# Three buffers for the stacked q and k operands, and the output's halves added on GpSimd

## The chip, the core and the metric

The kernel runs on one core of a Trainium2 chip. Its engines are TensorE (PE in the rows), VectorE (DVE), ScalarE (ACT), GpSimd (POOL) and SyncE (SP), which issues most DMAs; each works through its own list of instructions in order, and semaphores tie the lists together. The metric is the device time of one execution in microseconds (us), lower is better.

## The reference, cut to what matters

The whole computation is an attention with bucket masks, then a Fourier-mixing block with an MLP, then a second mixing block. The change touches the attention alone:

```python
B, H, S, D = q.shape                       # 2, 8, 768, 64
scale = 1.0 / np.sqrt(D)
q_bits = (np.einsum('bhsd,dk->bhsk', q, proj) > 0)   # 6 bits a row
k_bits = (np.einsum('bhsd,dk->bhsk', k, proj) > 0)
...
mask = q_bucket[:, :, :, None] == k_bucket[:, :, None, :]
scores = scale * np.matmul(q, k.transpose(0, 1, 3, 2))
scores = np.where(mask, scores, -1000000000.0)
attn = np.exp(scores - np.max(scores, axis=-1, keepdims=True))
attn = attn / (np.sum(attn, axis=-1, keepdims=True) + 1e-09)
return np.matmul(attn, v).astype(np.float32)
```

There are 16 heads (2 x 8) of 768 rows. Its output, laid out as 1,536 rows of 512, is the input X of the rest.

## The kernel before, in words

**Precision.** TensorE works in fp32r; for accuracy each operand is split into a high part (a rounded copy) and a low part (the rest), and products are made of them. For a head, QK holds q transposed in its upper 64 partitions and k transposed in its lower 64. `scale_q` (L492) multiplies the q half by 1/8 on GpSimd. `split_top` makes the stacked operands from it, also on GpSimd: TOPH, the high part (a cast, L500), and TOPL, the low part (a subtraction, L502). SyncE then moves pieces of them (`move_away`, L410 and L411; `move_in`, L417 and L418) so that TOPL, TOPH, QM and KM hold what the score products need.

**Bits and masks.** Six random projections give the bucket bits: unit "bits" of a head (L723 to L725, three matmuls for each half of 384 columns) needs TOPH and TOPL. ScalarE copies the signs out (MB, L642), GpSimd turns them into mask rows (MR, L507), and SyncE sends them into rows 64 to 75 of QM and KM (L426, L427), where the score product takes them as further terms.

**Slots.** The attention runs in slots, one for each of the 96 query tiles of 128 rows, 6 to a head. `schedule` writes the list, and every engine's program walks it. In slot n TensorE does, in this order: the scores of tile n (L770, L771); the transposes of the exponentials of tile n-2 (units eta and etb, L745, three transposes each); two of the six steps of the value product of the head before (L785, L786), whose third part ends a group of three tiles; and then the units of the slot. Those are: in slots 0 and 1 of head h the two "bits" units of head h+1, and in slots 3 and 5 the two "back" units of head h-1, which transpose its output (OS) back into rows (L756). VectorE takes the row maxima (L992) and the exponent's scale and bias (L995) and the low parts of the transposed exponentials (ETL, L1002); ScalarE takes the exponentials (E, L625), the high parts (ETH, L618) and the copies of the value product (OS, L634).

**Output.** A value product carries the high and the low part of v side by side, so that a "back" unit leaves 3 blocks of 128 columns whose two halves of 64 have to be added. ScalarE copies the second halves into OL2 (L647); VectorE adds a constant to the sums (L1022), takes the reciprocals (L1024), and adds the first halves from the bank to OL2 (L1028), all of this for each of the two units of a head. GpSimd's `finish` multiplies by the reciprocals into X (L515). A bank of the ring of three is free when the addition has run.

**GpSimd's order** is what the change moves. In the slots of head h its list holds: slot 0 `finish(h-2, 1)`; slot 1 `mask_rows(h+1)`; slot 2 `split_v(h+1)` (L531, L533), which waits until the value product of head h-1 has ended, then `scale_q(h+2)`; slot 3 `finish(h-1, 0)`; slot 5 `split_top(h+2)`. The "bits" of head h+2 come up on TensorE at the end of slot 0 of head h+1. In the first eight heads GpSimd also issues 16 DMAs for tables and weights, one in slot 2 and one in slot 4 (L560).

Of the kernel before, what the change touches and what calls it, by code (L numbers as in the profile page):

```python
# [5 lines left out]
F32 = mybir.dt.float32  # L6
# [5 lines left out]
P = 128  # L12
# [55 lines left out]
def program(nc, qk, v, projb, w1, w2, wth, wtr, wti, wch, ident_in, gamma_in, sign_in, cs_in, ss_in, alt_in, cd_in, sd_in, out):  # L68
# [35 lines left out]
    OL2 = put("OL2", [P, 2, HALF, D], F32, tail - 4 * 2 * DM)  # L104
    OS2 = put("OS2", [P, 2, HALF, D])
# [21 lines left out]
    XL = put("XL", [1, LC], F32R)  # L127
    used[0] = dft_at + 4 * 4 * QT * KC
# [6 lines left out]
    TOPH = put("TOPH", [P, 2, S], F32R)  # L135
    TOPL = put("TOPL", [P, 2, S], F32R)
# [58 lines left out]
    with ctx:  # L195
# [30 lines left out]
        for u in units:  # L226
# [22 lines left out]
                   "back": sem("s_sum")}  # L249
        s_ol = sem("s_ol")  # L250
# [137 lines left out]
        def _(sp):  # L388
# [16 lines left out]
            def move_away(h):  # L405
                b = h % 2
                sp.wait_ge(s_top, 2 * (h + 1))
                if h >= 2:
                    sp.wait_ge(s_s, QT * (h - 1))
                sp.dma_start(QM[0:D, b].bitcast(F32), TOPH[0:D, b].bitcast(F32)).then_inc(s_away, 16)  # L410
                sp.dma_start(KM[0:D, b].bitcast(F32), TOPL[D:P, b].bitcast(F32)).then_inc(s_away, 16)  # L411

            def move_in(h):
                b = h % 2
                sp.wait_ge(s_ring, done["bits", h, 1])
                sp.wait_ge(s_away, 32 * (h + 1))
                sp.dma_start(TOPL[D:P, b].bitcast(F32), QM[0:D, b].bitcast(F32)).then_inc(s_in, 16)  # L417
                sp.dma_start(TOPH[0:D, b].bitcast(F32), TOPH[D:P, b].bitcast(F32)).then_inc(s_in, 16)  # L418

# [55 lines left out]
        def _(pool):  # L475
# [18 lines left out]
            def split_top(h):  # L494
                b = h % 2
                pool.wait_ge(s_sq, h)
                pool.wait_ge(s_top, 2 * h)
                if h >= 2:
                    pool.wait_ge(s_s, QT * (h - 1))
                nc.gpsimd.tensor_copy(TOPH[:, b], QK[:, b]).then_inc(s_top, 1)  # L500
                pool.wait_ge(s_top, 2 * h + 1)
                nc.gpsimd.tensor_tensor(TOPL[:, b], QK[:, b], TOPH[:, b].bitcast(F32), ALU.subtract).then_inc(s_top, 1)  # L502
# [6 lines left out]
            def finish(h, i):  # L509
                first, half = h * QT + i * HALF, 2 * h + i  # L510
                st = slice(first % NSTAT, first % NSTAT + HALF)
                row = (h // H) * QT + i * HALF
                pool.wait_ge(s_inv, 2 * half + 2)
                pool.wait_ge(emptied["back"], half + 1)
                nc.gpsimd.tensor_tensor(X[:, row:row + HALF, (h % H) * D:(h % H + 1) * D], OS2[:, i],  # L515
# [22 lines left out]
            for slot, (tile, et, pv, us) in enumerate(slots):  # L538
# [15 lines left out]
                if slot and t == 3 and h:  # L554
                    finish(h - 1, 0)
                if slot and t == 5 and h + 2 < NH:
                    split_top(h + 2)
                if slot and t in (2, 4) and early:
# [33 lines left out]
        def _(act):  # L592
# [16 lines left out]
            for slot, (tile, et, pv, us) in enumerate(slots):  # L609
# [25 lines left out]
                for u in us:  # L635
# [7 lines left out]
                    elif kind == "back":  # L643
                        act.wait_ge(s_ring, done[u])
                        if h:
                            act.wait_ge(emptied["back"], nth[u] - 2)
                        nc.scalar.activation(OL2[:, i], blocks(ring(unit_no[u])[:, 0:HC])[:, :, D:P], ACT.Copy).then_inc(s_ol, 1)  # L647

# [71 lines left out]
        def _(pe):  # L720
# [12 lines left out]
            def unit(name):  # L733
# [12 lines left out]
                elif kind == "bits":  # L746
# [5 lines left out]
                    last = product(bank[0:2 * NM, 0:HC], projH[:], TOPH[:, h % 2, c], projL[:], TOPL[:, h % 2, c], True, True)  # L752
# [6 lines left out]
            for tile, et, pv, us in slots:  # L759
                if tile is not None:  # L760
# [7 lines left out]
                    for lo, hi in ((0, 512), (512, S)):  # L768
                        dst = s_bank(tile)[:, lo:hi]
                        nc.tensor.matmul(dst, TOPL[:, h % 2, c], TOPH[:, h % 2, lo:hi], start=True, stop=False)  # L770
# [170 lines left out]
        def _(dve):  # L941
# [44 lines left out]
            for slot, (tile, et, pv, us) in enumerate(slots):  # L986
# [23 lines left out]
                for u in us:  # L1010
# [234 lines left out]
```

## Time and profile before

| what | value |
|---|---|
| median of 3 runs | 849.54 us (846.16 to 853.26) |
| profiled execution | 848.04 us |
| its span | 845.3 us |
| mean granted TensorE clock | 0.96 |
| TensorE busy | 752.8 us (89%) |
| VectorE busy | 455.6 us (54%) |
| ScalarE busy | 318.4 us (38%) |
| GpSimd busy | 268.0 us (32%) |

The attention ends at about 315 us of the span. The page's line of slices (40 equal slices of 21 us) shows TensorE at 7 to 8 tenths there and at 9 after it, with a granted clock of 0.8 to 0.9 of full speed in most slices up to the eighth, and full speed from then to the end of the attention:

```profile
PE   3788888888888876979999999999997899999998
DVE  2667677778899987863221212121115656765433
POOL 2655555565656306734500000020001122321200
PEclk9889899999999997789999999999998999999999
```

The chain that ended last gives TensorE 75% of the span and GpSimd 12%; GpSimd's largest lines in it are L492 (4%) and L502 (3%).

### The profile page before, as it was taken

The numbers are of one execution on the slowest core, as the hardware profiler recorded it, in microseconds if no ns is written. First come the engines' busy times: TensorE is split into PE (matmuls) and PEld (weight loads), VectorE is DVE, ScalarE is ACT, GpSimd is POOL, SyncE is SP. The second block draws the span as 40 slices with busy tenths as digits, with TensorE's granted clock in tenths as the row PEclk, the third lists the DMA queues.
The fourth block names the chain that finished last, engine by engine and source line by source line (L and its number), as shares of the span: only waits on it lengthen the run. The fifth ranks groups of instructions, "written<-read, shape, count | busy, mean of one in ns | idle before, by whom it ended". The sixth has DMA issues, their size and how long they took to land.

```text
span 845.3 us, 11003 instructions
## 1 busy us (share of the span) xinstructions
PE 752.8 (89%) x3826; PEld 629.7 (74%) x3826; DVE 455.6 (54%) x834; ACT 318.4 (38%) x659; POOL 268.0 (32%) x243
## 2 busy tenths in 40 slices
PE   3788888888888876979999999999997899999998
PEld 2677777777877865768888888888885687888876
DVE  2667677778899987863221212121115656765433
ACT  2667667777877851111111111101113343231301
POOL 2655555565656306734500000020001122321200
PEclk9889899999999997789999999999998999999999
DMA  5343443553332103372200000220002222000001
GB/s 144 82 124 90 104 111 94 169 169 93 103 83 70 42 1 112 113 224 75 74 1 1 1 0 1 63 76 0 1 1 70 69 61 88 0 13 13 26 26 74
DMA packets 44680, 56.26 MB, mean 67 GB/s; under 512 B 15956, under 2 KB 27860, under 8 KB 44116
## 3 DMA queue, kind: packets, MB, share of 16 engines
q1 hardware_dynamic: 38100, 41.65, 17.8%
q0 software_dynamic: 6528, 13.92, 5.7%
q8 instruction: 32, 0.52, 0.3%
q14 instruction: 20, 0.16, 0.1%
HBM read 38.65 MB, written 3.15 MB: 49 GB/s over the span
## 4 chain that ended last, share of the span: by engine, by line
PE 75%; POOL 12%; DVE 5%; issue 3%; ACT 2%; DMA 1%; SPq 1%; POOLq 0%; ACTq 0%
PE PS L723 19%; PE PS L725 18%; PE PS L724 18%; PE PS L745 5%; POOL QK L492 4%; POOL TOPL L502 3%; PE PS L770 3%; PE PS L785 3%; PE PS L771 3%; PE PS L786 3%; POOL TOPH L500 1%; PE PS L906 1%; POOL VHL L531 1%; PE PS L913 1%; POOL VHL L533 1%
## 5 line engine op out<-in xcount | busy, mean ns | idle before, releaser
L1117 DVE SCALAR_TENSOR_TENSOR HL<-PS,HH 128x512 fp32r<-128x512 f32 x48 | 33.2, 692 | 186.6 <-ACT HH L686 186.6
L992 DVE TENSOR_REDUCE negmax<-PS 128x1 f32<-128x768 f32 x96 | 91.3, 951 | 59.9 <-PE PS L771 59.9
L625 ACT ACTIVATE E<-PS,affine 128x768 f32<-128x768 f32 x96 | 95.4, 994 | 39.7 <-DVE affine L995 38.2
L686 ACT ACTIVATE HH<-PS 128x512 fp32r<-128x512 f32 x48 | 28.7, 598 | 208.9 <-PE PS L725 208.9
L1002 DVE TENSOR_TENSOR ETL<-PS,ETH 128x384 fp32r<-128x384 f32 x192 | 97.9, 548 | 0.9 <-ACT ETH L618 0.5
L618 ACT ACTIVATE ETH<-PS 128x384 fp32r<-128x384 f32 x192 | 84.3, 489 | 24.5 <-PE PS L745 22.8
L745 PE MATMUL PS<-ident,E 128*128 128x128 f32 x576 | 84.5, 282 | 1.2
L785 PE MATMUL PS<-ETH,VHL 128*128 128x384 f32 x192 | 75.1, 391 | 8.9 <-ACT OS L634 6.3
L723 PE MATMUL PS<-UTH,W1H 128*128 128x512 f32 x192 | 76.2, 397 | 1.7 <-DVE UTL L1100 1.7
L770 PE MATMUL PS<-TOPH,TOPL 128*128 128x512 f32 x192 | 70.3, 366 | 6.7 <-DMA KM<-MR 6.0
L725 PE MATMUL PS<-UTH,W1L 128*128 128x512 f32 x192 | 75.3, 392 | 0.0
L724 PE MATMUL PS<-UTL,W1H 128*128 128x512 f32 x192 | 75.2, 392 | 0.0
L725 PE MATMUL PS<-W2H,HL 128*128 128x512 f32 x192 | 74.7, 389 | 0.0
L723 PE MATMUL PS<-W2H,HH 128*128 128x512 f32 x192 | 74.7, 389 | 0.0
L724 PE MATMUL PS<-W2L,HH 128*128 128x512 f32 x192 | 74.7, 389 | 0.0
L745 PEld LDWEIGHTS PS<-ident,E 128*128 128x128 f32 x576 | 68.2, 145 | 3.8 <-DVE ETL L1002 3.5
L507 POOL TENSOR_SCALAR MR<-MB,gamma 24x768 fp32r<-24x768 f32 x15 | 43.9, 2930 | 77.8 <-ACT MB L642 77.8
L786 PE MATMUL PS<-ETL,VHL 128*128 128x384 f32 x192 | 66.9, 348 | 0.0
L586 POOL TENSOR_TENSOR ZF<-X,SC 128x512 f32<-128x512 f32 x24 | 30.5, 1290 | 106.0 <-ACT SC L707 106.0
L771 PE MATMUL PS<-KM,QM 76*128 76x512 f32 x192 | 63.5, 351 | 0.0
L723 PE MATMUL PS<-ZH,WTH 128*128 128x512 f32 x144 | 59.2, 411 | 0.0
L725 PE MATMUL PS<-ZH,WTL 128*128 128x512 f32 x144 | 56.5, 392 | 0.0
(167 smaller groups left out, 1525.6 us busy)
## 6 DMA issues: line engine op xcount, KB each, us to landing
stage<-in_moe_w_ch_dram SPq DMA_DIRECT2D x36, 256.0 KB, 2.6
QK<-in_qk_dram SPq DMA_DIRECT2D x16, 384.0 KB, 3.9
W1H<-in_moe_w_ch_dram POOLq DMA_DIRECT2D x4, 1024.0 KB, 8.2
W2H<-in_moe_w_ch_dram POOLq DMA_DIRECT2D x4, 1024.0 KB, 8.9
QM<-TOPH SPq DMA_DIRECT2D x16, 192.0 KB, 2.8
KM<-TOPL SPq DMA_DIRECT2D x16, 192.0 KB, 3.1
TOPL<-QM SPq DMA_DIRECT2D x16, 192.0 KB, 2.7
TOPH<-TOPH SPq DMA_DIRECT2D x16, 192.0 KB, 3.0
```

The lines of the kernel that those rows point to most:

```text
L618: nc.scalar.activation(ETH[:, t // HALF, k * HALF:(k + 1) * HALF, (t % HALF) * P:(t % HALF + 1) * P], bank, ACT.Copy).then_inc(s_eth, 1)
L625: nc.scalar.activation(E[:, tile % NE, :], s_bank(tile)[:, 0:S], ACT.Exp, bias=affine[:, t, 1:2], scale=affine[:, t, 0:1], accum_out=esum[ ...
L723: nc.tensor.matmul(dst, hl, hr, start=start, stop=False)
L724: nc.tensor.matmul(dst, hl, lr, start=False, stop=False)
L725: return nc.tensor.matmul(dst, ll, hr, start=False, stop=stop)
L745: last = nc.tensor.transpose(bank[:, j * P:(j + 1) * P], E[:, tile % NE, (first + j) * P:(first + j + 1) * P], ident[:])
L770: nc.tensor.matmul(dst, TOPL[:, h % 2, c], TOPH[:, h % 2, lo:hi], start=True, stop=False)
L771: last = nc.tensor.matmul(dst, QM[:, h % 2, c], KM[:, h % 2, lo:hi], start=False, stop=True)
L785: nc.tensor.matmul(OT, VHL[:, h % 2, j, :], ETH[:, c, j, :], start=(j == 0), stop=False)
L786: last = nc.tensor.matmul(OT, VHL[:, h % 2, j, :], ETL[:, c, j, :], start=False, stop=(j == QT - 1))
L992: nc.vector.tensor_reduce(negmax[:, t, 1:2], s_bank(tile)[:, 0:S], AX_X, ALU.max, negate=True).then_inc(s_max, 1)
L1002: nc.vector.tensor_tensor(ETL[where], blocks(ring(unit_no[kind, h, t])[:, 0:HC]), ETH[where].bitcast(F32), ALU.subtract).then_inc(emptied[ ...
```

## The change

- TOPH and TOPL get a third buffer, and a head's parts are in buffer h % 3. `split_top(h)` on GpSimd then waits for the scores of head h-3 where it waited for those of head h-2. QK, QM and KM keep two.
- `split_top(h+2)` stands in slot 3 of head h where it stood in slot 5, and the second DMA of GpSimd in slot 5 where it stood in slot 4.
- ScalarE copies both halves of a "back" unit (128 x 384) into OL2, which sets the bank free.
- GpSimd adds the halves in `finish`, ahead of the multiplication, and waits for its own addition between them. VectorE's addition is gone.
- VectorE takes the reciprocals of a head's six columns at once, with the first "back" unit.

```diff
-    OL2 = put("OL2", [P, 2, HALF, D], F32, tail - 4 * 2 * DM)
-    OS2 = put("OS2", [P, 2, HALF, D])
+    OL2 = put("OL2", [P, 2, HALF, P], F32, tail - 4 * 2 * DM)
+    OS2 = put("OS2", [P, HALF, D])
...
             def move_away(h):
-                b = h % 2
+                b, r = h % 2, h % 3
                 sp.wait_ge(s_top, 2 * (h + 1))
                 if h >= 2:
                     sp.wait_ge(s_s, QT * (h - 1))
-                sp.dma_start(QM[0:D, b].bitcast(F32), TOPH[0:D, b].bitcast(F32)).then_inc(s_away, 16)
-                sp.dma_start(KM[0:D, b].bitcast(F32), TOPL[D:P, b].bitcast(F32)).then_inc(s_away, 16)
+                sp.dma_start(QM[0:D, b].bitcast(F32), TOPH[0:D, r].bitcast(F32)).then_inc(s_away, 16)
+                sp.dma_start(KM[0:D, b].bitcast(F32), TOPL[D:P, r].bitcast(F32)).then_inc(s_away, 16)
...
             def split_top(h):
-                b = h % 2
+                b, r = h % 2, h % 3
                 pool.wait_ge(s_sq, h)
                 pool.wait_ge(s_top, 2 * h)
-                if h >= 2:
-                    pool.wait_ge(s_s, QT * (h - 1))
-                nc.gpsimd.tensor_copy(TOPH[:, b], QK[:, b]).then_inc(s_top, 1)
+                if h >= 3:
+                    pool.wait_ge(s_s, QT * (h - 2))
+                nc.gpsimd.tensor_copy(TOPH[:, r], QK[:, b]).then_inc(s_top, 1)
                 pool.wait_ge(s_top, 2 * h + 1)
-                nc.gpsimd.tensor_tensor(TOPL[:, b], QK[:, b], TOPH[:, b].bitcast(F32), ALU.subtract).then_inc(s_top, 1)
+                nc.gpsimd.tensor_tensor(TOPL[:, r], QK[:, b], TOPH[:, r].bitcast(F32), ALU.subtract).then_inc(s_top, 1)
...
             def finish(h, i):
-                first, half = h * QT + i * HALF, 2 * h + i
-                st = slice(first % NSTAT, first % NSTAT + HALF)
+                half = 2 * h + i
+                st = slice((half * HALF) % NSTAT, (half * HALF) % NSTAT + HALF)
                 row = (h // H) * QT + i * HALF
-                pool.wait_ge(s_inv, 2 * half + 2)
                 pool.wait_ge(emptied["back"], half + 1)
-                nc.gpsimd.tensor_tensor(X[:, row:row + HALF, (h % H) * D:(h % H + 1) * D], OS2[:, i],
+                if half:
+                    pool.wait_ge(s_x, half)
+                nc.gpsimd.tensor_tensor(OS2[:], OL2[:, i, :, 0:D], OL2[:, i, :, D:P], ALU.add).then_inc(s_sum, 1)
+                pool.wait_ge(s_sum, half + 1)
+                pool.wait_ge(s_inv, 2 * (h + 1))
+                nc.gpsimd.tensor_tensor(X[:, row:row + HALF, (h % H) * D:(h % H + 1) * D], OS2[:],
                                         einv[:, st].unsqueeze(2).to_broadcast([P, HALF, D]), ALU.mult).then_inc(s_x, 1)
...
-                if slot and t == 3 and h:
-                    finish(h - 1, 0)
-                if slot and t == 5 and h + 2 < NH:
-                    split_top(h + 2)
-                if slot and t in (2, 4) and early:
+                if slot and t == 3:
+                    if h:
+                        finish(h - 1, 0)
+                    if h + 2 < NH:
+                        split_top(h + 2)
+                if slot and t in (2, 5) and early:
...
                         if h:
-                            act.wait_ge(emptied["back"], nth[u] - 2)
-                        nc.scalar.activation(OL2[:, i], blocks(ring(unit_no[u])[:, 0:HC])[:, :, D:P], ACT.Copy).then_inc(s_ol, 1)
+                            act.wait_ge(s_sum, nth[u] - 2)
+                        nc.scalar.activation(OL2[:, i], blocks(ring(unit_no[u])[:, 0:HC]), ACT.Copy).then_inc(emptied["back"], 1)
...
-                    elif kind == "back":
-                        first, half = h * QT + i * HALF, 2 * h + i
-                        st = slice(first % NSTAT, first % NSTAT + HALF)
-                        dve.wait_ge(s_exp, first + HALF)
+                    elif kind == "back" and i == 0:
+                        st = slice(h * QT % NSTAT, h * QT % NSTAT + QT)
+                        dve.wait_ge(s_exp, (h + 1) * QT)
                         nc.vector.tensor_scalar(einv[:, st], esum[:, st], 1e-9, None, ALU.add).then_inc(s_inv, 1)
-                        dve.wait_ge(s_inv, 2 * half + 1)
+                        dve.wait_ge(s_inv, 2 * h + 1)
                         nc.vector.reciprocal(einv[:, st], einv[:, st]).then_inc(s_inv, 1)
-                        dve.wait_ge(s_ol, nth[u])
-                        if h:
-                            dve.wait_ge(s_x, nth[u] - 2)
-                        nc.vector.tensor_tensor(OS2[:, i], blocks(bank[:, 0:HC])[:, :, 0:D], OL2[:, i], ALU.add).then_inc(emptied["back"], 1)
```

**GpSimd's list, one head.** From the split of v for head 2 to the first mask row after it, in head 1 of the attention. Before:

```order
L531 CAST VHL<-VR 128x6x64 [waits s_pv,s_v0]
L533 TENSOR_TENSOR VHL<-VR,VHL 128x6x64 [waits s_vs]
L492 TENSOR_SCALAR QK<-QK 64x768 [waits s_qk1]
L560 DMA CSH<-in_cs_dram 128x3x386
L515 TENSOR_TENSOR X<-OS_68,einv 128x3x64 [waits s_sum,s_inv]
L560 DMA SSH<-in_ss_dram 128x3x386
L500 CAST TOPH<-QK 128x768 [waits s_s,s_top,s_sq]
L502 TENSOR_TENSOR TOPL<-QK,TOPH 128x768 [waits s_top]
L515 TENSOR_TENSOR X<-OS_68,einv 128x3x64 [waits s_sum,s_inv]
L507 TENSOR_SCALAR MR<-MB,gamma 24x768 [waits s_mask,s_bits]
```

The same piece of the changed kernel (its lines are four or five further down):

```order
L535 CAST VHL<-VR 128x6x64 [waits s_pv,s_v0]
L537 TENSOR_TENSOR VHL<-VR,VHL 128x6x64 [waits s_vs]
L492 TENSOR_SCALAR QK<-QK 64x768 [waits s_qk1]
L565 DMA CSH<-in_cs_dram 128x3x386
L516 TENSOR_TENSOR OS_68<-OL_67 128x192 [waits s_ol]
L519 TENSOR_TENSOR X<-OS_68,einv 128x3x64 [waits s_inv,s_sum]
L500 CAST TOPH<-QK 128x768 [waits s_s,s_top,s_sq]
L502 TENSOR_TENSOR TOPL<-QK,TOPH 128x768 [waits s_top]
L565 DMA SSH<-in_ss_dram 128x3x386
L516 TENSOR_TENSOR OS_68<-OL_67 128x192 [waits s_x,s_ol]
```

The two instructions of `split_top` have the same neighbours as before but for two: the second DMA is behind them, and an addition (OS_68<-OL_67) stands ahead of them. In heads without DMAs the addition is the only difference.

**VectorE's list around the two "back" units of a head.** Before:

```order
L1002 TENSOR_TENSOR ETL<-PS,ETH 128x3x128 [waits s_eth] x2
L1022 TENSOR_SCALAR einv<-esum 128x3 [waits s_exp]
L1024 RECIPROCAL einv<-einv 128x3 [waits s_inv]
L1028 TENSOR_TENSOR OS_68<-PS,OL_67 128x192 [waits s_x,s_ol]
L992 TENSOR_REDUCE negmax<-PS 128x1 [waits s_s]
```

The changed kernel, at the first unit of a head:

```order
L1007 TENSOR_TENSOR ETL<-PS,ETH 128x3x128 [waits s_eth] x2
L1026 TENSOR_SCALAR einv<-esum 128x6 [waits s_exp]
L1028 RECIPROCAL einv<-einv 128x6 [waits s_inv]
L997 TENSOR_REDUCE negmax<-PS 128x1 [waits s_s]
L1000 SCALAR_TENSOR_TENSOR affine<-negmax 128x2 [waits s_max]
```

The addition and its wait for ScalarE are gone from in front of the row maximum; at the second unit nothing is left but the pair of ETL and the maximum.

## Rows read from the trace of the kernel before

**Rows 1.** Stretches from a head's bits to its v split: us, busy by engine, clock, DMA.

```profile
core 0: us, PE busy (x) PEld busy (x) DVE busy (x) ACT busy (x) POOL busy (x), PEclk, DMA share, GB/s
33.60:46.35 12.75, 12.75 (x67) 11.37 (x68) 7.87 (x17) 8.27 (x18) 2.93 (x1) 0.76 0.41 106
75.78:87.30 11.52, 11.52 (x67) 10.40 (x68) 7.73 (x17) 8.27 (x18) 3.25 (x2) 0.85 0.46 116
95.77:108.19 12.42, 12.42 (x67) 11.08 (x68) 7.87 (x17) 8.27 (x18) 3.25 (x3) 0.78 0.41 108
154.73:166.26 11.53, 11.53 (x67) 10.49 (x68) 7.86 (x17) 8.27 (x18) 3.25 (x2) 0.85 0.71 200
174.47:184.42 9.95, 9.95 (x67) 9.14 (x68) 7.71 (x16) 7.93 (x18) 3.25 (x2) 1.00 0.75 212
191.40:201.35 9.95, 9.95 (x67) 9.16 (x68) 8.53 (x18) 8.80 (x20) 3.25 (x2) 1.00 0.51 127
```

**Rows 2.** The same view, stretches from a v split to the next bits.

```profile
46.35:55.05 8.70, 4.58 (x32) 3.90 (x31) 6.07 (x14) 5.48 (x12) 8.50 (x9) 0.90 0.49 120
166.26:174.47 8.21, 4.57 (x32) 3.90 (x30) 6.09 (x14) 5.48 (x12) 8.01 (x9) 1.00 0.51 157
218.28:225.26 6.98, 4.79 (x31) 3.88 (x30) 6.78 (x14) 4.38 (x11) 6.81 (x7) 1.00 0.13 30
```

**Rows 3.** Timeline of GpSimd, a late head: start us, us, what [idle before <-releaser].

```profile
218.28 0.50 POOL L531 CAST VHL<-VR 128x384 fp32r<-128x384 f32 x1 [2.49 <-PE PS L786]
218.87 1.01 POOL L533 TENSOR_TENSOR VHL<-VR,VHL 128x384 fp32r<-128x384 f32 x1
219.85 2.13 POOL L492 TENSOR_SCALAR QK<-QK 64x768 f32<-64x768 f32 x1
221.96 0.50 POOL L515 TENSOR_TENSOR X<-OS,einv 128x192 f32<-128x192 f32 x1
222.42 0.81 POOL L500 CAST TOPH<-QK 128x768 fp32r<-128x768 f32 x1
223.31 1.80 POOL L502 TENSOR_TENSOR TOPL<-QK,TOPH 128x768 fp32r<-128x768 f32 x1
```

**Rows 4.** Timeline of GpSimd, a head with DMA issues.

```profile
170.56 0.52 POOL L515 TENSOR_TENSOR X<-OS,einv 128x192 f32<-128x192 f32 x1
171.01 0.59 POOL L560 DMA_DIRECT2D W1H<-in_moe_w_ch_dram  x1
171.60 0.84 POOL L500 CAST TOPH<-QK 128x768 fp32r<-128x768 f32 x1
```

**Rows 5.** Timeline of TensorE, instructions that end an idle time.

```profile
136.56 0.34 PE L723 MATMUL PS<-TOPH,projH 128*24 128x384 f32 x1 [3.17 <-POOL TOPL L502]
154.73 0.34 PE L723 MATMUL PS<-TOPH,projH 128*24 128x384 f32 x1 [2.73 <-POOL TOPL L502]
220.44 0.41 PE L785 MATMUL PS<-ETH,VHL 128*128 128x384 f32 x1 [0.57 <-ACT OS L634]
225.26 0.33 PE L723 MATMUL PS<-TOPH,projH 128*24 128x384 f32 x1 [1.49 <-POOL TOPL L502]
```

**Rows 6.** Timeline of VectorE and ScalarE around a "back" unit.

```profile
298.93 0.32 ACT L647 ACTIVATE OL<-PS 128x192 f32<-128x192 f32 x1
299.28 0.36 DVE L1028 TENSOR_TENSOR OS<-PS,OL 128x192 f32<-128x192 f32 x1 [0.15 <-ACT OL L647]
299.48 0.87 ACT L618 ACTIVATE ETH<-PS 128x384 fp32r<-128x384 f32 x2 [0.24 <-PE PS L745]
300.73 0.99 ACT L625 ACTIVATE E<-PS,affine 128x768 f32<-128x768 f32 x1 [0.37 <-DVE affine L995]
```

**Rows 7.** Timeline of VectorE beside the TOPL of Rows 3.

```profile
223.54 1.60 DVE L995 SCALAR_TENSOR_TENSOR affine<-negmax 128x2 f32<-128x2 f32 x1
```

**Rows 8.** Timeline of SyncE and TensorE: the mask rows of a head, and its first scores.

```profile
164.09 0.77 SPq L427 DMA_DIRECT2D KM<-MR  x1
...
169.02 0.48 PE L770 MATMUL PS<-TOPH,TOPL 128*128 128x512 f32 x1
```

**Rows 9.** The page's DMA issues: KB of each, median us to landing.

```profile
KM<-TOPL SPq DMA_DIRECT2D x16, 192.0 KB, 3.1
```

More of the change, by code:

```diff
@@ L127, in program @@
     XL = put("XL", [1, LC], F32R)
+    TOPL = put("TOPL", [P, 3, S], F32R)
     used[0] = dft_at + 4 * 4 * QT * KC
@@ L134, in program @@
     work_at = used[0]
-    TOPH = put("TOPH", [P, 2, S], F32R)
-    TOPL = put("TOPL", [P, 2, S], F32R)
+    TOPH = put("TOPH", [P, 3, S], F32R)
     QM = put("QM", [D + NM, 2, S], F32R)
@@ L248, in program @@
                    "pv": sem("s_os"),
-                   "back": sem("s_sum")}
-        s_ol = sem("s_ol")
+                   "back": sem("s_ol")}
+        s_sum = sem("s_sum")
         s_x = sem("s_x")
@@ L409, in move_away @@
                     sp.wait_ge(s_s, QT * (h - 1))
-                sp.dma_start(QM[0:D, b].bitcast(F32), TOPH[0:D, b].bitcast(F32)).then_inc(s_away, 16)
-                sp.dma_start(KM[0:D, b].bitcast(F32), TOPL[D:P, b].bitcast(F32)).then_inc(s_away, 16)
+                sp.dma_start(QM[0:D, b].bitcast(F32), TOPH[0:D, r].bitcast(F32)).then_inc(s_away, 16)
+                sp.dma_start(KM[0:D, b].bitcast(F32), TOPL[D:P, r].bitcast(F32)).then_inc(s_away, 16)
             def move_in(h):
-                b = h % 2
+                b, r = h % 2, h % 3
                 sp.wait_ge(s_ring, done["bits", h, 1])
                 sp.wait_ge(s_away, 32 * (h + 1))
-                sp.dma_start(TOPL[D:P, b].bitcast(F32), QM[0:D, b].bitcast(F32)).then_inc(s_in, 16)
-                sp.dma_start(TOPH[0:D, b].bitcast(F32), TOPH[D:P, b].bitcast(F32)).then_inc(s_in, 16)
+                sp.dma_start(TOPL[D:P, r].bitcast(F32), QM[0:D, b].bitcast(F32)).then_inc(s_in, 16)
+                sp.dma_start(TOPH[0:D, r].bitcast(F32), TOPH[D:P, r].bitcast(F32)).then_inc(s_in, 16)
             def move_mask(h):
@@ L494, in split_top @@
             def split_top(h):
-                b = h % 2
+                b, r = h % 2, h % 3
                 pool.wait_ge(s_sq, h)
                 pool.wait_ge(s_top, 2 * h)
-                if h >= 2:
-                    pool.wait_ge(s_s, QT * (h - 1))
-                nc.gpsimd.tensor_copy(TOPH[:, b], QK[:, b]).then_inc(s_top, 1)
+                if h >= 3:
+                    pool.wait_ge(s_s, QT * (h - 2))
+                nc.gpsimd.tensor_copy(TOPH[:, r], QK[:, b]).then_inc(s_top, 1)
                 pool.wait_ge(s_top, 2 * h + 1)
-                nc.gpsimd.tensor_tensor(TOPL[:, b], QK[:, b], TOPH[:, b].bitcast(F32), ALU.subtract).then_inc(s_top, 1)
+                nc.gpsimd.tensor_tensor(TOPL[:, r], QK[:, b], TOPH[:, r].bitcast(F32), ALU.subtract).then_inc(s_top, 1)
             def mask_rows(h):
@@ L751, in unit @@
                         pe.wait_ge(s_proj, 3)
-                    last = product(bank[0:2 * NM, 0:HC], projH[:], TOPH[:, h % 2, c], projL[:], TOPL[:, h % 2, c], True, True)
+                    last = product(bank[0:2 * NM, 0:HC], projH[:], TOPH[:, h % 3, c], projL[:], TOPL[:, h % 3, c], True, True)
                 elif kind == "back":
@@ L769, in _ @@
                         dst = s_bank(tile)[:, lo:hi]
-                        nc.tensor.matmul(dst, TOPL[:, h % 2, c], TOPH[:, h % 2, lo:hi], start=True, stop=False)
+                        nc.tensor.matmul(dst, TOPL[:, h % 3, c], TOPH[:, h % 3, lo:hi], start=True, stop=False)
                         last = nc.tensor.matmul(dst, QM[:, h % 2, c], KM[:, h % 2, lo:hi], start=False, stop=True)
```

## The prediction, as made before the changed kernel ran

> **What bounds the kernel now.** I read the page first, for the chain that ended last: outside the attention it is TensorE almost alone, and the change leaves that part as it is. Inside the attention GpSimd's L492 and L502 stand in it, so there TensorE waits for a slower partner. The timeline of GpSimd in a late head shows how. Its v split starts when TensorE's last value product of the head before has ended, after 2.49 us of waiting for it; then the split, the scaling (2.13), the multiplication into X (0.50), the cast to TOPH (0.81) and the subtraction to TOPL (1.80) follow without a break [rows 3]. TensorE's bits of the next head wait for TOPL: 1.49 us idle at 225.26 [rows 5]. So a head is a closed loop of two stretches, and I cut the trace at these two points with the view of busy time by stretch. From the bits to the v split TensorE is busy all the time, 9.95 us at a clock of 1.00 [rows 1]. From the v split to the bits GpSimd is busy for 6.81 of 6.98 us, and TensorE for 4.79 [rows 2]. The sum is 16.93 us, a late head's period. The reader is to see that only two things change a period: what GpSimd does in the second stretch, and TensorE's clock in the first.
>
> Both differ in the first eight heads. The second stretch takes 8.70 us in the first that has all its parts and 8.21 in the last; seven such stretches take 8.41 on average, since two DMA issues stand in them [rows 2, 4]. And the first stretch takes 9.95 us in two of these eight heads, 11.52 or 11.53 in three, and 12.3 to 12.8 in three, at mean clocks of 0.85 and 0.76 to 0.79 [rows 1]: the granted clock fell to the lower of its two levels, 1.2 GHz, after TensorE had stood idle. Above 9.95 the eight add up to 12.4 us. An idle time of 2.73 us was followed by a fall (the stretch from 154.73, clock 0.85), one of 3.17 was not, and one of 1.49 was not [rows 1, 5].
>
> **The third buffer and the earlier slot.** They remove a wait of `split_top` for scores of the head before the last. That wait is not what holds it: the cast starts the moment the multiplication ahead of it has ended, with no idle time on GpSimd [rows 3]. In GpSimd's list `split_top` keeps its place behind the v split and the scaling, so "two heads ahead" is what it was before. It still cannot start before the last value product of the head before. Worth nothing by itself; what hides it is the list's order. SyncE's moves wait for TOPL and for QM and KM, which keep two buffers, and so stay where TOPL puts them.
>
> **The second DMA behind TOPL.** This one is off the loop now. The two issues cost 8.41 - 6.98 = 1.43 us, one half 0.71 (the issue itself shows 0.59 [rows 4]). Seven heads give 5.0 us, and the first head another 0.5: **-5.5 us**. Behind TOPL it fills time in which GpSimd waits for its mask rows anyway.
>
> **The addition on GpSimd.** The first `finish` of a head stands in the second stretch, ahead of TOPH and TOPL. The nearest rows for its addition (two inputs in SBUF, 128 x 192) are the multiplication of the same size, 0.50, and half of the 128 x 384 subtraction, 0.50 [rows 3]. The multiplication now waits for it, and where one GpSimd instruction waits for another's result the rows show 0.08 us between them (218.78 to 218.87, 223.23 to 223.31). So 0.58 us; the bounds are 0.36, VectorE's time for the same addition [rows 6], and 1.01, should it cost what twice the size does. Thirteen stretches have it (seven with DMAs, six without): 13 x 0.58 = **+7.5 us**, with bounds of 4.7 and 13. The second `finish` runs behind TOPL, in idle time, and costs nothing. The Trainium skill, "GPSIMD Engine Reference", section "Engine selection", speaks against the move: it wants elementwise work with two inputs on VectorE and calls GpSimd about twice as slow. By that factor on VectorE's 0.36 the addition would take 0.72 and the sum would be 2 us higher; here the same-sized row of 0.50 decides.
>
> **VectorE's relief.** In slots 3 and 5 the row maximum no longer stands behind the addition, which ended at 299.64 and held the maximum up. The exponential after it then goes when ScalarE is free, at the end of ETH (299.48 + 0.87 = 300.35) where it went at 300.73: 0.38 us earlier [rows 6]. ScalarE's longer copy (about 0.48 for 128 x 384, where it was 0.32) still ends before that ETH starts. The copy OS and the value product behind it come 0.38 earlier, so that TensorE's idle of 0.57 [rows 5] shrinks to some 0.2. But inside the loop this shortens nothing: TensorE merely reaches the wait for TOPL sooner. Only the last two heads, which have no split left to wait for, gain it: 2 x 0.38, less 0.15 for the longer copy at the end: **-0.6 us**. The reciprocals once a head are in the same place, off the path.
>
> **The clock.** The wait for TOPL grows. In the six late heads it was 1.49; it becomes 1.49 + 0.58 + 0.38 = 2.45 us. No row shows such a length. Of the neighbours, 1.49 never cost the clock, 2.73 did once, 3.17 did not once. So bound it by no fall and six falls, and take three, because 2.45 is nearer to 2.73 and even longer gaps were let off. A fall costs 11.53 - 9.95 = 1.58 us [rows 1]: **+4.7 us**, with bounds of 0 and 9.5. In the early heads the gap is 0.13 shorter by GpSimd and 0.38 longer by VectorE's relief; I take half a fall more than now, **+0.8**. The Trainium skill, "TensorE: Matmul & The Clock Gate", section "Why this matters for your kernels", has a rule of thumb by which idle gaps of 2.45 us would be harmless; by it the two clock terms would be nothing. The trace's fall after 2.73 us is against it, and that is the first rival.
>
> **A port.** VectorE's small L995 took 1.60 us beside GpSimd's TOPL, and ended with it [rows 7], where it takes 0.16 alone. The Trainium skill, "SBUF — State Buffer", section "Who interferes with whom", calls that an exclusive lock of the two engines. The addition brings more of it, but it falls into the stretch where TensorE waits for TOPL in any case, so I cost it at nothing.
>
> **The sum** is made against the profiled execution, 848.04 us, which is 1.5 below the median: 848.0 - 5.5 + 7.5 - 0.6 = 849.4 without the clock, and + 4.7 + 0.8 = **855 us**. About 1% (8.5 us) is what a measurement of this kernel can tell from no change: up to 858.0 and down to 841.0.
>
> **The rivals.**
> - *The clock stays up* in the late heads, or falls once: 849.4 to 851, no change. For it: 3.17 us was let off. Against it: 2.73 was not. Chance 0.25.
> - *The clock falls in five or six late heads, and in all early ones*: 849.4 + 9.5 + 2 x 1.6 to 2 x 2.5, or 862 to 864; with an addition of nearly 1.01 us, 868. For it: six of eight early gaps were followed by a fall. Chance 0.18.
> - *The other side: the early heads keep their clock.* The issue that leaves the loop is worth up to 0.8 us in the heads with the large tables, and if the addition took only 0.36, the early gaps would shrink by 0.3 to 0.4. Should that let all six early falls go, while 2.3 us in the late heads is harmless, the time would be 849.4 - 2.8 - 12.4 = 834; with four of the six gone 838. It decides from early gaps of under 2.7 us, and these stand at 2.73 to 3.65. Chance 0.06.
> - *A late DMA.* The second weight transfer (1 MB) goes out behind TOPL, together with SyncE's moves. The mask rows of a head were issued until 164.86 and the scores that need them started at 169.02 [rows 8], 4.2 us for a transfer of some 3.1 us [rows 9]. If the moves come 3 us later in two or three heads, TensorE waits some 2 us in each and the clock may fall as well: 859 to 861. Chance 0.04.
> - The forecast, two to four falls in the late heads, 852 to 858: chance 0.47.
>
> **How the numbers follow.** The likeliest is 855. The range runs from 848, which takes in the case of no fall with a cheaper addition, to 864, which takes in most of the case of all falls. Slower by over 1%: 0.18 + 0.04 and a fifth of the forecast's own 0.47 at its upper end, 0.31. Faster by over 1%: 0.06 and 0.01 for what is not thought of: 0.07. The rest, 0.62, is within 1%.
>
> **What would show it.** In the profile after: the stretch from the v split to the bits at 7.56 us in late heads and about 8.3 in early ones; L516 at 0.50 ahead of each TOPH; TensorE's wait for TOPL near 2.4 us; the value product of slot 5 waiting 0.2 instead of 0.57; first stretches of 11.5 us among the late heads, where there were none. The prediction is wrong if GpSimd idles ahead of TOPH in the trace of before after all (it does not in these rows), if the late period falls below 16.9 us, or if the time after the attention differs.

## The result: 2.7% slower

The changed kernel took 870.58 us (median of 4 runs, 868.66 to 876.39) against 847.85 us of the kernel before on the same chip (4 runs, 844.84 to 853.26): a ratio of 1.0272, with an interval of [1.0196, 1.0348]. The forecast was 855 us with a range up to 864. The profiled execution took 868.66 us, its span 866.6 us, its mean granted clock 0.933 where it had been 0.96.

The stretches of the changed kernel, cut as in [rows 1]: from a head's bits to the next v split. The first four are early heads, the others late ones.

```profile
core 0: us, PE busy (x) PEld busy (x) DVE busy (x) ACT busy (x) POOL busy (x), PEclk, DMA share, GB/s
32.42:44.97 12.55, 12.55 (x67) 11.20 (x68) 8.00 (x17) 8.71 (x19) 3.29 (x3) 0.77 0.41 105
74.30:85.84 11.54, 11.54 (x67) 10.47 (x68) 7.92 (x17) 8.70 (x19) 4.46 (x4) 0.85 0.51 127
135.63:147.12 11.49, 11.49 (x67) 10.38 (x68) 7.84 (x17) 8.70 (x19) 4.45 (x5) 0.85 0.54 128
176.22:188.60 12.38, 12.38 (x67) 11.06 (x68) 8.02 (x17) 8.69 (x19) 4.43 (x4) 0.79 0.74 185
...
196.29:206.23 9.94, 9.94 (x67) 9.14 (x68) 7.85 (x17) 8.13 (x19) 3.84 (x4) 1.00 0.52 127
...
231.45:243.00 11.55, 11.55 (x67) 10.47 (x68) 8.02 (x17) 8.70 (x19) 3.84 (x4) 0.85 0.45 114
...
250.67:263.33 12.66, 12.66 (x67) 11.31 (x68) 8.01 (x17) 8.70 (x19) 3.84 (x3) 0.77 0.40 105
...
291.36:304.15 12.79, 12.79 (x67) 11.38 (x68) 8.01 (x17) 8.69 (x19) 3.84 (x3) 0.76 0.28 67
```

No early stretch is at 9.95 us any more: two of the eight read 11.5 us and six read 12.2 to 12.6 (all eight add up to 97.5 us, where it was 92.0). Of the six late ones, which all read 9.95 before, one reads 11.55 and three 12.66 to 12.79. The number of instructions (x67 on TensorE) is the same; only the clock (0.76 to 0.85) differs.

The stretches from a v split to the next bits, which answer to [rows 2]:

```profile
core 0: us, PE busy (x) PEld busy (x) DVE busy (x) ACT busy (x) POOL busy (x), PEclk, DMA share, GB/s
44.97:53.52 8.55, 4.58 (x31) 3.90 (x30) 5.36 (x10) 5.15 (x12) 8.28 (x9) 0.90 0.34 89
167.93:176.22 8.29, 4.58 (x32) 3.90 (x30) 5.78 (x10) 5.27 (x12) 8.02 (x9) 0.91 0.45 145
206.23:213.88 7.65, 4.57 (x32) 3.90 (x31) 5.56 (x10) 5.45 (x12) 7.41 (x8) 1.00 0.12 29
263.33:270.98 7.65, 4.59 (x32) 3.91 (x31) 5.70 (x10) 5.26 (x12) 7.40 (x8) 0.95 0.08 19
```

In early heads GpSimd's stretch is what it was (8.39 on average, where it was 8.41), in late ones it is 7.65 where it was 6.98. In the last row the clock is already down inside the gap (0.95 on average; in steps of 1 us it reads 1.00 up to 270 us and 0.64 from 270 to 271, the last step before the bits). GpSimd's timeline of a late head, against [rows 3]:

```profile
206.23 0.50 POOL L535 CAST VHL<-VR 128x384 fp32r<-128x384 f32 x1 [2.47 <-PE PS L791]
206.81 1.00 POOL L537 TENSOR_TENSOR VHL<-VR,VHL 128x384 fp32r<-128x384 f32 x1
207.79 2.14 POOL L492 TENSOR_SCALAR QK<-QK 64x768 f32<-64x768 f32 x1
209.91 0.59 POOL L516 TENSOR_TENSOR OS<-OL 128x192 f32<-128x192 f32 x1
210.58 0.51 POOL L519 TENSOR_TENSOR X<-OS,einv 128x192 f32<-128x192 f32 x1
211.03 0.82 POOL L500 CAST TOPH<-QK 128x768 fp32r<-128x768 f32 x1
211.93 1.80 POOL L502 TENSOR_TENSOR TOPL<-QK,TOPH 128x768 fp32r<-128x768 f32 x1
```

The chain is the old one with L516 in it, 0.67 us from its start to the multiplication's. On TensorE, against [rows 5], the value product of slot 5 hardly waits, and the wait for TOPL has nearly doubled:

```profile
207.71 0.41 PE L790 MATMUL PS<-ETH,VHL 128*128 128x384 f32 x1 [0.24 <-ACT OS L639]
213.88 0.33 PE L728 MATMUL PS<-TOPH,projH 128*24 128x384 f32 x1 [2.83 <-POOL TOPL L502]
250.67 0.49 PE L728 MATMUL PS<-TOPH,projH 128*24 128x384 f32 x1 [3.00 <-POOL TOPL L502]
```

The spans differ by 21.3 us (866.6 and 845.3). Summed over the stretches of the two profiles:

| part | difference, us | forecast |
|---|---|---|
| up to the first v split, and the first head's short stretch | -1.2 | -0.5 |
| v split to bits, seven early | -0.2 | -0.9 |
| v split to bits, six late | +4.1 | +3.5 |
| bits to v split, eight early (clock) | +5.5 | +0.8 |
| bits to v split, six late (clock) | +9.9 | +4.7 |
| last value products of the attention | -0.9 | -0.6 |
| behind the attention | +4.1 | 0 |

The last row is mostly the clock as well. I read the granted clock behind the last value product in steps of 2 us: the time at the lower level adds up to 37.5 us in the kernel before and to 44.4 in the changed one. By TensorE's busy time in those steps that is some 3.7 of the 4.1 us, an estimate.

### The profile page after: what moved, and what is told of

It is laid out like the page before. It is cut to its first block, busy times and chain, and to the rows that moved or that the text cites. A ratio compares the mean times of both kernels' runs of the same rounds, so it can differ in the third digit from the quotient of the medians.

```text
span 866.6 us, 10972 instructions
## 1 busy us (share of the span) xinstructions
PE 769.5 (89%) x3826; PEld 644.4 (74%) x3826; DVE 440.3 (51%) x770; ACT 325.2 (38%) x659; POOL 287.5 (33%) x275
## 4 chain that ended last, share of the span: by engine, by line
PE 77%; POOL 12%; DVE 4%; issue 3%; DMA 1%; ACT 1%; SPq 1%; POOLq 0%; ACTq 0%
PE PS L728 19%; PE PS L729 18%; PE PS L730 18%; PE PS L750 6%; POOL QK L492 3%; PE PS L775 3%; PE PS L790 3%; PE PS L776 3%; PE PS L791 3%; POOL TOPL L502 3%; POOL TOPH L500 1%; PE PS L911 1%; POOL OS L516 1%; POOL VHL L535 1%; PE PS L918 1%
## 5 line engine op out<-in xcount | busy, mean ns | idle before, releaser
L750 PE MATMUL PS<-ident,E 128*128 128x128 f32 x576 | 86.9, 290 | 0.1
L790 PE MATMUL PS<-ETH,VHL 128*128 128x384 f32 x192 | 77.6, 404 | 2.6 <-ACT OS L639 1.2
L775 PE MATMUL PS<-TOPH,TOPL 128*128 128x512 f32 x192 | 72.9, 380 | 7.0 <-DMA KM<-MR 6.0
L750 PEld LDWEIGHTS PS<-ident,E 128*128 128x128 f32 x576 | 71.6, 149 | 1.1 <-DVE ETL L1007 0.8
L791 PE MATMUL PS<-ETL,VHL 128*128 128x384 f32 x192 | 69.1, 360 | 0.0
L776 PE MATMUL PS<-KM,QM 76*128 76x512 f32 x192 | 65.9, 362 | 0.0
L728 PE MATMUL PS<-TOPH,projH 128*24 128x384 f32 x32 | 14.8, 462 | 52.6 <-POOL TOPL L502 46.7
```

The costliest lines, as they stand in the source:

```text
L728: nc.tensor.matmul(dst, hl, hr, start=start, stop=False)
L750: last = nc.tensor.transpose(bank[:, j * P:(j + 1) * P], E[:, tile % NE, (first + j) * P:(first + j + 1) * P], ident[:])
L775: nc.tensor.matmul(dst, TOPL[:, h % 3, c], TOPH[:, h % 3, lo:hi], start=True, stop=False)
L776: last = nc.tensor.matmul(dst, QM[:, h % 2, c], KM[:, h % 2, lo:hi], start=False, stop=True)
L790: nc.tensor.matmul(OT, VHL[:, h % 2, j, :], ETH[:, c, j, :], start=(j == 0), stop=False)
L791: last = nc.tensor.matmul(OT, VHL[:, h % 2, j, :], ETL[:, c, j, :], start=False, stop=(j == QT - 1))
```

## The experiments

Each was timed in three rounds (seven to nineteen runs of the kernel before beside it). The theory: GpSimd's list sets the loop, and the idle time it leaves TensorE lowers the granted clock, which is most of the loss. The rival: the work itself, the port or the new buffers cost the time. The kernel before was timed beside each group of experiments, and its median was 847.4 to 850.4 us; so kernels of different groups are better compared by their ratios to it.

**Keep TensorE busy in the gap.** Two kernels, the changed one and the one before (there with `% 2`), with `K` matmuls of no use:

```diff
                 elif kind == "bits":
                     c = slice(i * HC, (i + 1) * HC)
+                    if h >= 2 and i == 0:
+                        for _ in range(K):
+                            nc.tensor.matmul(bank[0:2 * NM, 0:HC], projH[:], TOPH[:, (h - 1) % 3, 0:HC], start=True, stop=True)
                     pe.wait_ge(s_top, 2 * (h + 1))
```

> The changed kernel with matmuls of no use ahead of TensorE's wait for TOPL (16 in the eight heads with DMAs, 12 in the late ones; each 128*24 by 384, written to the bits' bank, which the bits then overwrite). Clock theory: most of the loss is the granted clock. No first stretch (bits to v split) is over 10.1 us, the clock in them 1.00; the second stretches stay at 8.3 to 8.5 and 7.65, since GpSimd sets their length; 15.5 us for the eight early and 9.9 us for the six late stretches come back: about 841 to 846 us, faster than the kernel before. Rival, that the falls are not caused by the idle time, or that the longer GpSimd list is the whole loss: the falls stay or go over to another place, and the time stays at 865 to 870 us.

> The kernel before with the same kind of matmuls (14 in the early heads, 6 in the late ones). Clock theory: the six falls of the early heads (12.4 us over eight stretches) go, nothing else changes: 834 to 838 us. The difference between this kernel and the changed one with its filler is then the change without its clock: the second stretches (+4.1 late, -0.7 early), start and end (-1.5), +1 to +4 us. Rival (the change costs much more than these stretches): a difference of over 8 us stays between the two.

Measured: 840.86 us for the changed kernel (ratio to the kernel before 0.9913 [0.9876, 0.9950]) and 835.90 us for the kernel before (0.9868 [0.9822, 0.9913]). So with 200 matmuls more (16 in each of eight heads, 12 in each of six), the changed kernel is 30 us faster than without them; the kernel before gains 12 with 148 (14 and 6). Here a first stretch begins with the first of these matmuls. An early and a late head of the changed kernel with them:

```profile
core 0: us, PE busy (x) PEld busy (x) DVE busy (x) ACT busy (x) POOL busy (x), PEclk, DMA share, GB/s
156.89:170.38 13.49, 12.91 (x84) 10.70 (x83) 9.03 (x20) 9.25 (x22) 7.92 (x9) 1.00 0.85 229
170.38:175.04 4.66, 4.41 (x31) 3.95 (x30) 4.42 (x8) 4.33 (x10) 4.50 (x5) 1.00 0.41 101
...
227.71:240.60 12.89, 12.22 (x80) 10.28 (x79) 8.98 (x20) 9.26 (x22) 6.79 (x6) 1.00 0.39 98
240.60:245.26 4.66, 4.42 (x31) 3.96 (x30) 4.42 (x8) 4.33 (x10) 4.49 (x5) 1.00 0.19 44
```

The clock is 1.00 in every stretch of the attention, in both kernels. The late head takes 12.89 + 4.66 = 17.55 us, which is what the changed kernel's takes where its clock does not fall (7.65 + 9.94): the matmuls fill the gap and do not shorten GpSimd's list. What is left between the two kernels with the clock out of the way is 840.86 - 835.90 = 5.0 us, a little above the 1 to 4 expected and far from the rival's 8 or more; the late heads' 0.67 us, six times, would be 4.0 of it. The two profiles are 8.5 us apart, of which 3.2 lie ahead of the last v split (275.68 and 272.49) and 5.3 behind it. So of the 23 us of the loss some 18 go with the clock in the attention, counting what it costs either kernel.

**One more addition on GpSimd, VectorE's left in place.** The kernel before, with an addition of 128 x 192 whose result nobody reads:

```diff
                 pool.wait_ge(emptied["back"], half + 1)
+                if i == 0:
+                    if h:
+                        pool.wait_ge(s_dum, h)
+                    nc.gpsimd.tensor_tensor(DUM[:], OS2[:, i], OS2[:, i], ALU.add).then_inc(s_dum, 1)
+                    pool.wait_ge(s_dum, h + 1)
```

> The kernel before with one more addition of 128x192 on GpSimd ahead of each head's first multiplication, with its wait; its result is not used. VectorE's addition stays. Theory: the late second stretch goes from 6.98 to 7.6 us, the late gap to 1.49+0.6 = 2.1 us (the value product keeps its 0.57 of waiting), the early gaps to 3.3 to 4.2. If the length of the gap decides on the clock, the late heads at 2.1 us lose it less often than those of the changed kernel at 2.9 (0 to 3 of 6, one of them 1.6 us), the early ones all: 13*0.6 = 8 us, +3 to 6 us for the early clock, +0 to 5 for the late one: 859 to 867 us. Rival (the addition is the whole loss, and VectorE's relief has no part in it): the late heads fall as often as in the changed kernel, 4 of 6, most of them for 2.4 us or more: 868 us or more.

Measured: 866.56 us (860.21 to 873.52), 1.0204 [1.0130, 1.0277]. The late stretch from v split to bits is 7.56 us, the gaps of the late heads 2.05 to 2.51 us, and two of the six late heads lose the clock, by 1.6 us each, where the changed kernel loses it in four and for longer. This profile is of the fastest of the four runs, so the others may have lost it more often. The early heads lose it in all eight, as expected, but after gaps of 3.2 to 4.2 us they lose only 1.5 to 1.6 each, 12.5 in all, where it was 12.4 before and 3 to 6 more were expected. So the addition in the loop makes a loss of 2% by itself, 19 of 23 us, though this kernel lacks the gain of the second DMA that the changed one has. By the medians it is 4 us better than the changed kernel, but the intervals overlap; that VectorE's relief makes matters worse shows in the gaps (2.1 to 2.5 against 2.8 to 3.0) and is not clear in the time.

**The addition back on VectorE**, all else as changed:

```diff
-                nc.gpsimd.tensor_tensor(OS2[:], OL2[:, i, :, 0:D], OL2[:, i, :, D:P], ALU.add).then_inc(s_sum, 1)
...
+                        nc.vector.tensor_tensor(OS2[:, i], blocks(bank[:, 0:HC])[:, :, 0:D], OL2[:, i], ALU.add).then_inc(emptied["back"], 1)
```

> The changed kernel with the addition back on VectorE and the narrow copy on ScalarE; the third buffer, the second DMA behind TOPL and the reciprocals once a head stay. Theory: the late second stretches are 6.98 again, the early ones 7.7 (8.41 less 0.7), gaps of about 1.5 to 1.7 in the late heads and 2.2 to 3.0 in the early ones, so that the early falls get fewer: 848 - 5.5 - 0 to 9 = 833 to 843 us. Rival (the third buffer or its place in memory costs something by itself): 850 us or more.

Measured: 838.04 us, 0.9883 [0.9833, 0.9933]. The rest of the change is a gain of 1.2%, so the addition's move costs 3.9% (1.0272 against 0.9883).

**The second DMA behind `split_top`, alone**, in the kernel before:

```diff
-                if slot and t in (2, 4) and early:
+                if slot and t in (2, 5) and early:
```

> The kernel before with the second DMA of a head on GpSimd behind split_top, and nothing else. Theory: early second stretches 7.7 in place of 8.4 us, five and a half us in all, early gaps 2.1 to 3.0 us and fewer falls, 0 to 9 us more: 833 to 843 us, about as e4_after_dve_add, so the third buffer adds nothing to it. Rival (this part of the change is worthless because the transfer comes late): 846 us or more.

Measured: 839.29 us, 0.9886 [0.9824, 0.9948]: the same as the one above, whose profiled stretches it repeats to 0.05 us. So the third buffer and the reciprocals once a head add nothing to it.

**The first `finish` of a head behind `split_top`**, the addition staying on GpSimd:

```diff
                 if slot and t == 3:
-                    if h:
-                        finish(h - 1, 0)
                     if h + 2 < NH:
                         split_top(h + 2)
+                    if h:
+                        finish(h - 1, 0)
```

> The changed kernel with the first finish of a head (addition and multiplication) behind split_top. Theory: 1.07 us leave the loop: late second stretch 7.65-1.07 = 6.58 us, early 7.25, gaps of 1.9 us in late and 2.2 to 2.5 us in early heads; no or few falls: 828 to 842 us. Rival (the addition costs by its port or its work, wherever it stands): 860 us or more.

Measured: 841.10 us, 0.9872 [0.9814, 0.9929]. The late second stretch is 6.62 us. The same addition on the same engine, off the loop, leaves the time at what it is with the addition on VectorE (0.9883). The multiplication left the loop with it, so this does not show that the addition alone costs nothing there. Six of the fourteen heads still lost the clock, two of them late heads after gaps of 1.95 and 1.80 us, which was not expected; the other four late heads kept it after 1.82 to 1.96.

**The length of the gap.** The changed kernel with fewer of the matmuls: `K` of 4 and of 8 in each of the fourteen heads.

> The changed kernel with 4 matmuls of no use ahead of TensorE's wait for TOPL in every head: gaps of 2.9-0.7 = 2.2 us in late heads and 2.9 to 3.2 in early ones; GpSimd's list as in the changed kernel. Theory (the length of the gap sets how often and how long the clock falls): the three falls of 2.7 us in late heads turn into shorter or no falls (0 to 5 us in the six in place of 9.9), the early ones shrink from 17.9 to about 12 us as in the kernel before: 853 to 862 us. Rival (filler of any length does it, or the falls have another cause): 841 to 846 as with 12 to 16 matmuls, or 868 and more.

> The same with 8 matmuls: gaps of 1.5 us in late heads, as in the kernel before, and 2.2 to 2.5 us in early ones. Theory: no falls in the late heads, 2 to 5 single ones in the early heads (0 to 8 us): 842 to 851 us. Rival: the late heads keep falls although their gap is that of the kernel before: 853 us or more.

Measured: 850.35 us (ten runs, 1.0032 [0.9998, 1.0066]) and 847.97 us (ten runs, 0.9974 [0.9935, 1.0013]). The first is 3 us better than expected. The six late heads of six profiles, by the idle time of TensorE ahead of the bits:

| gap of the late heads, us | kernel | heads with a fall | us lost in the six |
|---|---|---|---|
| 0.9 to 1.4 | changed, 8 matmuls | 0 | 0 |
| 1.49 | before | 0 | 0 |
| 1.8 to 2.0 | `finish` behind | 2 | 3.2 |
| 2.0 to 2.2 | changed, 4 matmuls | 2 | 3.1 |
| 2.1 to 2.5 | before, one more addition | 2 | 3.2 |
| 2.8 to 3.0 | changed | 4 | 9.9 |

Longer gaps in the late heads go with more falls, but within one profile the length does not decide: with one more addition the two falls stand behind gaps of 2.05 and 2.06 us, and the two gaps of 2.5 were let off. Nor does it set the price of a fall. In the eight early heads, by the same cut:

| gap of the early heads, us | kernel | heads with a fall | us of one fall |
|---|---|---|---|
| 1.2 to 2.4 | changed, 8 matmuls | 5 | 1.5 to 1.6 |
| 1.9 to 3.1 | changed, 4 matmuls | 5 | 1.6 |
| 2.7 to 3.65 | before | 6 | 1.6 in three, 2.4 to 2.8 in three |
| 3.1 to 3.9 | changed | 8 | 1.5 to 1.6 in two, 2.3 to 2.6 in six |
| 3.2 to 4.2 | before, one more addition | 8 | 1.5 to 1.6 |

The early falls with 4 matmuls cost some 8 us together where about 12 were expected, which accounts for the 3 us by which that kernel was faster than forecast. The profile with 8 matmuls is of one of its longer runs (853.66 us).

**The split ahead of the v split.** Here the three buffers are put to use: in the changed kernel, `scale_q` and `split_top` no longer stand behind the wait for the value product.

```diff
-                    if h + 1 < NH:
-                        split_v(h + 1)
                     if h + 2 < NH:
                         scale_q(h + 2)
+                        split_top(h + 2)
+                    if h + 1 < NH:
+                        split_v(h + 1)
                 if slot and t == 3:
                     if h:
                         finish(h - 1, 0)
-                    if h + 2 < NH:
-                        split_top(h + 2)
```

> The changed kernel with scale_q and split_top of head h+2 moved ahead of split_v(h+1) on GpSimd, so that they no longer wait for the value product of the head before; this is where three buffers allow the parts two heads ahead. Theory of the loop: TOPL of the next head is there before TensorE gets to its bits, TensorE has no wait of over 1 us in the heads, the second stretch falls to TensorE's own 4.8 to 5.2 us and the clock is 1.00: per head 9.95+5.0 = 15 us for 14 heads, some 14*1.9 + 9*0.5 (early DMAs) + 12 = 43 us under the kernel before: 800 to 812 us. Rival (a next wait stands right behind: mask rows or the DMAs of the moves): a new idle time of 1 us or more at L770/L775, 815 to 840 us.

Measured: **800.84 us, 0.9410 [0.9365, 0.9455]**, faster than both kernels. GpSimd's timeline of a late head:

```profile
199.18 2.93 POOL L507 TENSOR_SCALAR MR<-MB,gamma 24x768 fp32r<-24x768 f32 x1 [2.70 <-ACT MB L646]
202.09 2.13 POOL L492 TENSOR_SCALAR QK<-QK 64x768 f32<-64x768 f32 x1
204.29 0.82 POOL L500 CAST TOPH<-QK 128x768 fp32r<-128x768 f32 x1
205.20 1.83 POOL L502 TENSOR_TENSOR TOPL<-QK,TOPH 128x768 fp32r<-128x768 f32 x1
206.98 0.50 POOL L535 CAST VHL<-VR 128x384 fp32r<-128x384 f32 x1
```

The scaling and the split to TOPH and TOPL now follow the mask rows in time in which GpSimd used to wait for the value product, and TOPL is done at 207.03, as the v split starts and 2.2 us ahead of the bits at 209.24. One whole head, v split to v split, in this kernel:

```profile
core 0: us, PE busy (x) PEld busy (x) DVE busy (x) ACT busy (x) POOL busy (x), PEclk, DMA share, GB/s
207.00:221.62 14.62, 14.41 (x98) 13.13 (x97) 13.27 (x28) 13.40 (x30) 11.36 (x12) 1.00 0.39 100
```

TensorE is busy for 14.41 of 14.62 us; the period was 16.93 before and 17.6 to 20.4 in the changed kernel. One early head of this profile takes 17.24 us: VectorE's small L999 takes 1.69 us there (from 129.72) and ends with TOPL at 131.4, and TensorE waits 1.35 us for the ETL behind it, against the expectation of no wait over 1 us.

**The same with two buffers** (`h % 2`, and the wait of the kernel before):

> As e5_split_first, but with two buffers for TOPH and TOPL, so that the cast waits for the last scores of the head before. Theory: the scaling is done early, cast and subtraction (2.7 us) start at the end of slot 5's scores and end about 1 us before the bits: nearly the same as e5, 800 to 815 us, so the order and not the third buffer is what matters. Rival: the wait for the scores binds and the gap before the bits stays at 1 us or more, and the v split behind it comes late: 820 us or more.

Measured: 809.06 us, 0.9506 [0.9462, 0.9551]; the third buffer is worth 8 us here. No wait for TOPL is left, as expected. But the cast now waits for the last scores, TOPL falls beside slot 5, and VectorE's small L999 is held until TOPL has ended (215.71), as L995 was in [rows 7], now with TensorE behind it:

```profile
213.90 1.83 DVE L999 SCALAR_TENSOR_TENSOR affine<-negmax 128x2 f32<-128x2 f32 x1
215.66 1.01 DVE L1006 TENSOR_TENSOR ETL<-PS,ETH 128x384 fp32r<-128x384 f32 x2
```

```profile
213.88 1.83 POOL L502 TENSOR_TENSOR TOPL<-QK,TOPH 128x768 fp32r<-128x768 f32 x1
```

```profile
216.25 1.01 PE L749 MATMUL PS<-ident,E 128*128 128x128 f32 x6 [0.57 <-DVE ETL L1006]
```

A head takes 15.52 us, 0.9 more than with three buffers; this wait is 0.57 of it, and the rest was not followed. The order without the third buffer brings 41 us against the kernel before (the GpSimd addition and the DMA's place are in these 41), the third buffer another 8.

The lock between the two engines is what the Trainium skill, "SBUF — State Buffer", section "Who interferes with whom", states as a rule; the trace agrees, with 1.83 us for an instruction on two elements a partition.

**The addition on VectorE once the loop is gone:**

> e5_split_first with the addition back on VectorE (narrow copy on ScalarE, reciprocals once a head). Theory: with the split out of the loop GpSimd has time to spare (11 of 14.6 us) while VectorE has not (it was busy for 13.3 of 14.6 us), so here the addition is better on GpSimd: VectorE's list grows by 2*0.36 us and its waits for ScalarE, and the period by 0 to 0.7 us: 801 to 811 us. Rival (the engine of the addition does not matter): 801 us as e5.

Measured: 805.84 us, 0.9503 [0.9456, 0.9549], 5 us slower by the medians than with the addition on GpSimd, and 8 by the ratios (0.9503 against 0.9410), since the two were timed in different groups. In every head the value product waits 0.57 us for OS again, and a head takes 15.3 us:

```profile
core 0: us, PE busy (x) PEld busy (x) DVE busy (x) ACT busy (x) POOL busy (x), PEclk, DMA share, GB/s
195.99:211.31 15.32, 14.62 (x97) 13.11 (x97) 13.82 (x29) 13.29 (x32) 10.15 (x9) 1.00 0.38 97
```

**The changed kernel once more**, unchanged:

> The changed kernel once more, unchanged, with its own profile. Theory: the second stretches repeat to 0.1 us (8.3 to 8.5 early, 7.65 late); the falls in the late heads come in another pattern, 3 to 6 of them, together 5 to 13 us; the time after the attention is 559 to 566 us, differing from the first profile by the clock alone. Rival (a cause of the change itself behind the attention): again 3 us more than the 559.3 of the kernel before, with the same clock.

Measured: 869.77 us, 1.0243 [1.0186, 1.0301]. The second stretches repeat. Against the expectation the falls repeat too, head by head; what varies is the time behind the attention, 565.8 us from the last v split where it was 562.5 in the first profile of the same kernel and 559.3 in the kernel before. The time at the lower clock behind the last value product adds up to 51.2 us here, where it was 44.4 and 37.5. So differences of 3 us in that part come without any change, by the clock. That the +4.1 of the table has nothing to do with the change is not shown by this: both profiles of the changed kernel lie above the kernel before, as the rival had it, though not at the same clock. In the profiles of the experiments that part took 560.8 us or more wherever GpSimd did the addition, and 559.4 to 559.9 in three of the five where it did not (the other two 562.3 and 563.8). The cause stays open.

## Why the prediction was wrong, by its own steps

- **What bounds the kernel** was right: the loop of two stretches, with GpSimd's list in one and TensorE's clock in the other, is what every experiment moved.
- **The third buffer is worth nothing by itself** was right (the DMA alone does the same as the DMA, the buffer and the reciprocals together), and so was its reason: `split_top` stands behind a v split that waits. Lifted over it, the buffer is worth 8 us.
- **The second DMA** was forecast at -5.5 us. The table has -0.2 for seven early stretches, out of this gain and the additions; moved alone in the kernel before, the DMA took 0.6 to 0.8 us from each, and with three early falls fewer it came to 1.1%.
- **The addition** was forecast at 0.58 us and measured 0.67 (0.59 and the wait): +4.1 us for +3.5 in the late heads. A small miss; its row was another instruction of the same size.
- **VectorE's relief** was forecast at 0.38 us and was about 0.7. I counted the wait for OS, which shrank from 0.57 to 0.24, and missed the transposes of slot 5: the six ahead of that value product take 0.82 us where the same six took 1.18, and TensorE's busy time of the stretch fell from 4.79 to 4.57 with the same work. Before, and in the changed kernel:

```profile
218.69 1.18 PE L745 MATMUL PS<-ident,E 128*128 128x128 f32 x6
206.65 0.82 PE L750 MATMUL PS<-ident,E 128*128 128x128 f32 x6
```

- **The clock** is the step that failed. The gap of the six late heads was to grow from 1.49 to 2.45 us; it became 2.8 to 3.0. The price of a fall, 11.53 - 9.95 = 1.58 us, took the cheapest of the rows: [rows 1] also had 12.42 and 12.75, 2.5 and 2.8 us above 9.95, and three of the four late falls cost 2.7 to 2.85 and six of the eight early ones 2.3 to 2.6. The number of falls was close in the late heads (three forecast, four measured) and too low in the early ones, where half a fall more was forecast and two more came, with the others dearer: +5.5 us for +0.8. The two clock terms were forecast at 5.5 us and measured 15.4. The rival of five or six falls was priced with 1.58 as well and so ended at 864, too low.
- **The time behind the attention** was put at no difference, and a difference was named as a sign of being wrong. It came: +4.1 us, most of it at the lower clock. The prediction looked for falls in the heads alone.
- **Off the path** was right for the port in the changed kernel: TensorE is busy for all of the 9.94 us behind the bits. With two buffers and the split ahead, the same lock stands on the path.

What stays open: why gaps of equal length cost the clock in one head and not in the next, and why one fall costs 1.6 us and another 2.8. The pattern repeats between two profiles of one kernel, so it is not chance alone; nothing here shows what sets it.

## What to carry to other kernels

Before an instruction is moved to the engine with the lowest busy share, look whether that engine's list is what the critical one waits for at that place: GpSimd was busy for 32% of the span and for 98% of the stretch that mattered. A wait of the tensor engine should be priced with what it does to the clock of the work behind it, by all the rows that show a fall, the dear ones too, and relief on another engine that only brings TensorE to its wait sooner makes the wait longer. And a buffer more brings something only if the instruction that fills it does not stand behind a wait for something else.

## What the runs showed of the hardware

Gaps of 1.8 to 2.0 us already cost TensorE's clock in two of six heads, and gaps of 2.8 to 3.0 us in four of six. A fall cost 1.5 to 1.6 us or 2.3 to 2.85 us of the work behind it, and the length of the gap does not tell which: gaps of 3.2 to 4.2 us cost 1.5 to 1.6 in all eight heads of one profile, gaps of 2.96 to 3.00 cost 2.7 to 2.85 in three heads of another. With 200 useless matmuls in the gaps the clock read 1.00 in the whole attention, and the changed kernel was 30 us faster. The Trainium skill, "TensorE: Matmul & The Clock Gate", section "Why this matters for your kernels", has a rule of thumb by which gaps of 1.8 to 2.5 us would be harmless; the falls after such gaps (e.g. 1.80 and 2.06 us) are against it, and the measurement decides.
